# Spreading softmax sums over partitions by a DRAM round trip instead of wide transposes

## The reference, cut to what matters

```python
def _attn_ref(q, k, v, n_sink, window):          # 2 x 8 heads, 768 tokens, head_dim 64
    scores = scale * np.matmul(q, k.transpose(0, 1, 3, 2))
    keep = is_sink | in_window                   # 4 sinks, window 128
    scores = np.where(keep, scores, -1000000000.0)
    scores = scores - np.max(scores, axis=-1, keepdims=True)
    a = np.exp(scores)
    a = a / (np.sum(a, axis=-1, keepdims=True) + 1e-09)
    return np.matmul(a, v).astype(np.float32)
...
    x = np.ascontiguousarray(attn_out.transpose(0, 2, 1, 3)).reshape(B * S, H * D)
    x = _moe_ref(x=x, **moe_kwargs)              # silu(x w_gate) * (x w_val), times w_out
    return _moe2_ref(x=x, **moe2_kwargs)         # 8 experts, one for each token, skip gate
```

## Time and profile before

| | |
|---|---|
| median of 3 runs | 565.16 us (563.53 to 565.97) |
| the profiled execution | 564.08 us |
| its span, first to last instruction | 562.4 us |
| mean granted TensorE clock | 0.997 of 2.4 GHz |
| PE busy over the span | 545.3 us (97%) |
| attention, first instruction to the first product of the dense layer | 85.0 us |
| first 20 us to 40 us: PE, DVE, ACT, POOL busy | 20.00, 15.28, 14.55, 7.28 us |

### The profile page before, as it was taken

One profiled execution on the slowest core, in us unless ns is written; L12 is line 12 of the kernel. 1 busy time (PEld: TensorE's weight loads), 2 busy tenths in 40 slices (PEclk: granted clock), 3 DMA queues, 4 the chain that ended last, 5 costly groups with the idle time before them and its releaser, 6 DMA issues.

```text
span 562.4 us, 10755 instructions
## 1 busy us (share of the span) xinstructions
PE 545.3 (97%) x3830; PEld 454.0 (81%) x3830; DVE 237.4 (42%) x666; ACT 177.0 (31%) x421; POOL 102.6 (18%) x161
## 2 busy tenths in 40 slices
PE   7999999999999999999999999999989999999993
PEld 5777777888888888888888888888778888888882
DVE  5777771332323333232332444633641452445141
ACT  5777762121111212111133424322410330343030
POOL 7234457201111110100000010010211111111111
PEclk9999999999999999999999999999999999999998
DMA  8988522110011111000062112761267588396110
GB/s 234 276 272 233 163 80 79 57 56 21 36 56 56 56 56 56 0 0 1 0 249 106 56 53 74 276 251 57 100 200 273 187 331 314 123 332 228 43 29 28
DMA packets 28935, 71.67 MB, mean 127 GB/s; under 512 B 2833, under 2 KB 15121, under 8 KB 24801
## 3 DMA queue, kind: packets, MB, share of 16 engines
q1 hardware_dynamic: 25808, 62.82, 33.0%
q0 software_dynamic: 2560, 8.09, 4.5%
q10 hardware_dynamic: 528, 0.26, 0.2%
HBM read 61.11 MB, written 10.05 MB: 127 GB/s over the span
## 4 chain that ended last, share of the span: by engine, by line
PE 93%; DMA 2%; issue 1%; DVE 1%; POOL 1%; ACT 1%; POOLq 0%; DVEq 0%
PE bank L1518 13%; PE bank L1317 12%; PE bank L1315 12%; PE bank L1313 12%; PE bank L1390 6%; PE bank L1394 6%; PE bank L1392 6%; PE bank L1299 4%; PE bank L1530 4%; PE bank L1532 4%; PE bank L1531 4%; PE bank L1276 3%; PE bank L1255 3%; PE bank L1410 2%; PE bank L1269 1%
## 5 line engine op out<-in xcount | busy, mean ns | idle before, releaser
L1313 PE MATMUL bank<-x_hi,w_hi 128*128 128x512 f32 x288 | 112.2, 390 | 0.6 <-issue 0.6
L1317 PE MATMUL bank<-x_hi,w_lo 128*128 128x512 f32 x288 | 112.1, 389 | 0.0
L1315 PE MATMUL bank<-x_lo,w_hi 128*128 128x512 f32 x288 | 112.0, 389 | 0.0
L1518 PEld LDWEIGHTS bank<-xgT,w_sb 128*128 128x128 f32 x704 | 80.2, 192 | 2.3 <-issue 1.1
L1518 PE MATMUL bank<-xgT,w_sb 128*128 128x96 f32 x704 | 80.2, 275 | 1.0 <-ACT xgT L857 1.0
L1031 DVE TENSOR_TENSOR sig<-sig,bank 128x512 f32<-128x512 f32 x36 | 24.8, 688 | 128.1 <-ACT sig L759 128.1
L759 ACT ACTIVATE sig<-bank 128x512 f32<-128x512 f32 x36 | 21.5, 598 | 159.7 <-PE bank L1317 159.7
L1313 PEld LDWEIGHTS bank<-x_hi,w_hi 128*128 128x128 f32 x288 | 54.1, 188 | 12.2 <-issue 1.0
L1315 PEld LDWEIGHTS bank<-x_lo,w_hi 128*128 128x128 f32 x288 | 54.1, 188 | 11.3
L1317 PEld LDWEIGHTS bank<-x_hi,w_lo 128*128 128x128 f32 x288 | 54.0, 188 | 11.1
L1390 PE MATMUL bank<-wo_hi,hh_hi 128*128 128x512 f32 x132 | 53.6, 406 | 0.0
(11 more groups left out here) (173 smaller groups left out, 748.0 us busy)
## 6 DMA issues: line engine op xcount, KB each, us to landing
w_raw<-w SPq DMA_DIRECT2D x16, 1024.0 KB
w_sb<-w SPq DMA_DIRECT2D x16, 1024.0 KB, 7.6
w_raw<-w_gv SPq DMA_DIRECT2D x12, 512.0 KB, 3.5
va_sb<-v_long SPq DMA_DIRECT2D x10, 512.0 KB, 4.0
vb_sb<-v_tail SPq DMA_DIRECT2D x10, 320.0 KB, 5.6
k_sb<-kT SPq DMA_DIRECT2D x12, 256.0 KB, 6.2
wo_raw<-w_out SPq DMA_DIRECT2D x12, 256.0 KB, 3.6
out<-x SPq DMA_DIRECT2D x12, 256.0 KB, 2.1
```

The costliest lines, as they stand in the source:

```text
L1313: nc.tensor.matmul(ps[:, :], w_hi[:, u, a, k, :], x_hi[:, k, tok], start=(k == 0), stop=False)
L1315: nc.tensor.matmul(ps[:, :], w_hi[:, u, a, k, :], x_lo[:, k, tok], start=False, stop=False)
L1317: last = nc.tensor.matmul(ps[:, :], w_lo[:, u, a, k, :], x_hi[:, k, tok], start=False, stop=(k == KD - 1))
L1518: last = nc.tensor.matmul(ps, w1_sb[u][:, k, fc], xgT[:, k * ET:k * ET + ET], start=(k == 0), stop=(k == KD - 1))
```

## The change

The reciprocals stay 128x8. PE transposes them once into 8 partitions x 128 (8 rows of weights, one matmul). ACT copies that into `rsumT`. SP writes it to a DRAM tensor `sum_rows` and waits for it, and then reads it back with two transfers, each spreading 4 rows (2 KB) over 64 partitions, into `rbc_sb`, which has two halves now. X waits for these transfers (`rbc_in`). POOL's widening is gone. In the list, R moves from group B (after V of h 3) to group A (after its two T), X from group A to the group B that follows it, and Q from group A to the end of the group B before it. SP's `spread_sums(tile - 3)` stands between the loads of columns and of values.

```diff
--- before.py
+++ after.py
@@ -64,7 +64,7 @@
         for n in (g, g + 1):
             if n < PAIRS:
                 steps.append(("S", n // HP, n % HP, n))
-        for n in (g - 7, g - 6):
+        for n in (g - 9, g - 8):
             if 0 <= n < PAIRS and n % HP == HP - 1:
                 steps.append(("X", n // HP, None, n // HP))
         for n in (g - 3, g - 2):
@@ -72,17 +72,17 @@
                 steps.append(("T", n // HP, n % HP, psum_use))
                 turned[psum_use] = n
                 psum_use += 1
-                if n % HP == HP - 1:
-                    steps.append(("Q", n // HP, None, n // HP))
+        if g >= HP and (g - 3) % HP == HP - 1 and g - 3 < PAIRS:
+            steps.append(("R", (g - 3) // HP, None, psum_use))
+            psum_use += 1
         for n in (g - 5, g - 4):
             if 0 <= n < PAIRS:
                 tile, hp = divmod(n, HP)
                 steps.append(("V", tile, hp, None))
-                if hp == HP - 1:
-                    steps.append(("R", tile, None, psum_use))
-                    psum_use += 1
                 if tile in EARLY and hp == 1:
                     steps.append(("W", tile, None, tile - EARLY[0]))
+        if 0 < g <= PAIRS and (g - 1) % HP == HP - 1:
+            steps.append(("Q", (g - 1) // HP, None, (g - 1) // HP))
     v_use = itertools.count()
     return [(k, t, h, next(v_use)) if k == "V" else (k, t, h, n) for k, t, h, n in steps], turned
 
@@ -110,6 +110,7 @@
             return ctx.enter_context(nc.semaphore(name))
 
         expert_rows = nc.dram_tensor("expert_rows", (TRASH + P, ROW), F32).ap()
+        sum_rows = nc.dram_tensor("sum_rows", (NT, H, P), F32).ap()
 
 
         base = -(-nc.sbuf_base // 64) * 64
@@ -128,8 +129,8 @@
         scores_sb = place("scores_sb", (P, 4, SC), 0, 50.75)
         probsT = place("probsT", (P, TURNED, 4 * P), 0, 54.5)
         xT = place("xT", (P, 2, DM), 2, 0)
-        rbc_sb = place("rbc_sb", (P, DM), 2, 4)
-        rsum_wide = place("rsum_wide", (P, DM), 2, 6)
+        rbc_sb = place("rbc_sb", (P, 2, DM), 2, 4)
+        rsumT = place("rsumT", (P, 2, P), 2, 17)
         h_sb = place("h_sb", (P, NT, FT1, P), 0, 0)
 
 
@@ -275,7 +276,8 @@
         probs_ready = sem("probs_ready")
         pT_in_psum = sem("pT_in_psum")
         pT_by_act, pT_by_dve = sem("pT_by_act"), sem("pT_by_dve")
-        rsum_ready, rsum_spread = sem("rsum_ready"), sem("rsum_spread")
+        rsum_ready, rsum_out = sem("rsum_ready"), sem("rsum_out")
+        rbc_in = [sem("rbc_in0"), sem("rbc_in1")]
         pv_done = sem("pv_done")
         sums_step = sem("sums_step")
         silu_step = sem("silu_step")
@@ -401,16 +403,33 @@
                     sp.dma_start(va_sb[:, tile % 3, :, :], va[b, t - 1, :, :, :]).then_inc(v_in[t], 16)
                     sp.dma_start(vb_sb[0:TAIL, tile % 3, :, :], vb[b, t - 1, :, :, :]).then_inc(v_in[t], 16)
 
+            def spread_sums(tile):
+                use = next(n for kind, t, _, n in ORDER if kind == "R" and t == tile)
+                sp.wait_ge(pT_by_act, evacuated(use)[1])
+                sp.dma_start(sum_rows[tile, :, :], rsumT[0:H, tile % 2, :]).then_inc(rsum_out, 16)
+                sp.wait_ge(rsum_out, tile * 16 + 16)
+                if tile >= 2:
+
+                    sp.wait_ge(o_ready, tile - 1)
+                for u in range(2):
+                    sp.dma_start(rbc_sb[u * D:u * D + D, tile % 2, :],
+                                 sum_rows[tile, u * HP:u * HP + HP, :].rearrange("h q -> (h q)").unsqueeze(0)
+                                 .broadcast_to([D, DM])).then_inc(rbc_in[tile % 2], 16)
+
             load_columns(0)
             for tile in range(NT):
                 if tile + 1 < NT:
                     load_columns(tile + 1)
+                if tile >= 3:
+                    spread_sums(tile - 3)
                 load_values(tile)
                 if tile == QT - 1:
                     for f in range(2):
                         sp.dma_start(w_raw[:, f, :, :, :], w_gv[f, :, :, :, :]).then_inc(w_in[f], 16)
                         sp.dma_start(wo_raw[:, f, :], w_out[f, :, :]).then_inc(wo_in[f], 16)
                     sp.dma_start(wr_sb[:, :, :], w_route).then_inc(wr_in, 16)
+            for tile in range(NT - 3, NT):
+                spread_sums(tile)
             with if_wide(sp):
                 with sp.Fori(0, B) as b:
                     with sp.Fori(0, HP) as hp:
@@ -608,16 +627,11 @@
             make_mask(0)
             find_wide()
             for tile in range(NT):
-                if tile == QT - 1:
+                if tile == QT - 3:
                     copy_sinks(1)
-                pool.wait_ge(rsum_ready, tile + 1)
-                nc.gpsimd.tensor_copy(rsum_wide.rearrange("p (h c) -> p h c", h=H),
-                                      rsum[:, tile % 2, :].unsqueeze(2).broadcast_to([P, H, D])).then_inc(rsum_spread, 1)
-                if tile:
-                    split_x(tile - 1)
-                    if tile - 1 in EARLY:
-                        split_w(tile - 1 - EARLY[0])
-            split_x(NT - 1)
+                split_x(tile)
+                if tile in EARLY:
+                    split_w(tile - EARLY[0])
 
             with pool.Fori(0, FT1 // 2) as j:
                 for u in range(2):
@@ -726,9 +740,11 @@
                                          ).then_inc(pT_by_act, 1)
                 elif kind == "R":
                     a.wait_ge(pT_in_psum, n + 1)
-                    if tile:
-                        a.wait_ge(o_ready, tile)
-                    nc.scalar.activation(rbc_sb, pT_ps[n % 2][:, :], ACT.Copy).then_inc(pT_by_act, 1)
+                    if tile >= 2:
+
+                        a.wait_ge(rsum_out, (tile - 1) * 16)
+                    nc.scalar.activation(rsumT[0:H, tile % 2, :], pT_ps[n % 2][0:H, 0:P], ACT.Copy
+                                         ).then_inc(pT_by_act, 1)
                 elif kind == "W":
                     split_half(n // 2, n % 2, 16)
 
@@ -951,18 +967,18 @@
                                           ).then_inc(pT_by_dve, 1)
                 elif kind == "Q":
                     d.wait_ge(probs_ready, tile * H + H)
-                    nc.vector.tensor_scalar(rsum[:, tile % 2, :], sums[:, qt % 2, :], 1e-9, None, ALU.add
+                    nc.vector.tensor_scalar(rsum[:, tile % 2, :].rearrange("p (u h) -> p h u", u=2),
+                                            sums[:, qt % 2, :].rearrange("p (h u) -> p h u", u=2), 1e-9, None, ALU.add
                                             ).then_inc(sums_step, 1)
                     d.wait_ge(sums_step, tile + 1)
                     nc.vector.reciprocal(rsum[:, tile % 2, :], rsum[:, tile % 2, :]).then_inc(rsum_ready, 1)
                 elif kind == "X":
-                    use = next(m for k, t, _, m in ORDER if k == "R" and t == tile)
                     d.wait_ge(pv_done, LAST_V[tile] + 1)
-                    d.wait_ge(pT_by_act, evacuated(use)[1])
+                    d.wait_ge(rbc_in[tile % 2], tile // 2 * 32 + 32)
                     if tile >= 2:
 
                         d.wait_ge(xT_ready, tile - 1)
-                    nc.vector.tensor_tensor(xT[:, tile % 2, :], o_ps[tile % 2][:, :], rbc_sb, ALU.mult
+                    nc.vector.tensor_tensor(xT[:, tile % 2, :], o_ps[tile % 2][:, :], rbc_sb[:, tile % 2, :], ALU.mult
                                             ).then_inc(o_ready, 1)
 
             with if_wide(d):
@@ -1264,10 +1280,8 @@
                         by_act, count = evacuated(n - 2)
                         pe.wait_ge(pT_by_act if by_act else pT_by_dve, count)
                     if kind == "R":
-                        pe.wait_ge(rsum_spread, tile + 1)
-                        for hp in range(HP):
-                            last = nc.tensor.transpose(pT_ps[n % 2][:, hp * P:hp * P + P],
-                                                       rsum_wide[:, hp * P:hp * P + P], ident[:, :])
+                        pe.wait_ge(rsum_ready, tile + 1)
+                        last = nc.tensor.transpose(pT_ps[n % 2][0:H, 0:P], rsum[:, tile % 2, :], ident[:, :])
                     else:
                         pe.wait_ge(probs_ready, tile * H + h * 2 + 2)
                         for u in range(2):
```

## The result

The changed kernel takes 594.28 us (median of 4 runs, 592.10 to 594.98), the kernel before 564.91 beside it. The ratio is 1.0527, 95% interval 1.0503 to 1.0551. The direction was forecast, the size was not: 579.0 was the number, 573 to 587 its range.

A forecast was written before the change was run, and what follows sets the result against it. PE was taken as the bound, busy all of 20 us in attention. Tiles' extra times, mainly R waiting for ACT's copy, summed to 14.1 us on 564.08, giving 578.2 (579.2 beside the median), range 573 to 587.

The forecast's parts named there:

- R's wait for ACT: In group A, PE's R waits for ACT's copy of h 3, ending 3.45 us in; group A takes 4.79 instead of 2.97.
- the sum: Over attention, the changes in tile times add up to 14.1 us more, giving 578.2, or 579.2 beside the median.
- The saving of 0.4 us for the single transpose: On PE, R falls from 0.59 to 0.2 us, giving back 0.4 us a tile, 4.8 us by itself.
- Q and X move on DVE into group B: DVE ends 4.02 us after group B's start, shifting the chain to ACT's copy by 0.25; group A takes 5.04 us.
- the paragraph on POOL: POOL is busy 7.28 of 20 us and nobody waits for its copy, so removing it is worth nothing.
- 0 to 4 us there and take 0: At tile 3, the sums' write queues behind tile 5's values and 1.5 MB of weights; cost put at 0.
- The rival that put the whole trip late: SP's chain of write, reads and loads sets the pace, 7.5 to 9 us a tile, about 586; 25 in 100.
- The end: After the last R, the trip takes 9.2 to 10.3 us against 11.8 available: hidden, 1.5 us to spare.
- the rival with the shorter chain: R waits, but DVE's shift is 0 and X hidden; a tile pays 1.1 us, about 575; 15 in 100.
- From there everything is shifted and nothing is longer: Sign to look for: first dense product comes at 99, and everything behind it is only shifted.

The follow-up runs named there:

- The order alone: Kernel before with the changed kernel's attention order, double rbc_sb, but still four transposes and POOL's spreading copy, no DRAM trip: 584.48 us, ratio 1.0353.
- the last variant: Kernel before, without DRAM trip, with R at the head of group A, Q in group B before the copies, X in group A: 566.83 us, ratio 1.0039.

## Why the forecast was right in direction and half in size

The step that was to decide, R's wait for ACT, came as forecast. Three terms of the sum failed: Q on DVE was priced at 0.32 us and took 1.11, the clock behind R's wait had no term, and the DRAM trip was taken at 0 and cost 3 to 5 us.

**What PE waits for: right.** R in group A waits 11 times for ACT's copy of h 3. The order alone gives a tile of 8.08 us against 8.17 and 14.0 us against the sum's 14.1, and moving the copy to DVE takes 10.8 us of it away. The saving of 0.4 us for the single transpose holds too: 0.20 in place of 0.59.

**"Q and X move on DVE into group B": mis-sized.** The term priced Q at 0.32 us from the earlier trace rows. It measured 1.11. R's waits add up to 21.5 us, against 17.8 where the order stands alone and Q is short: 3.7 us. The mistake is in the paragraph on POOL: "the removal is worth nothing". POOL's copy had waited for Q and kept `x_lo` behind it. Moving Q brought DVE and POOL together, and removing the copy took the guard away. The Trainium skill (SBUF — State Buffer, SBUF: two separate sides) says that DVE and GpSimd share one pair of ports, an exclusive lock that a GpSimd instruction, or a DVE instruction in a mode with two ports, holds for its whole length, so that the other blocks. The trace agrees for Q's first half, which ends with POOL's subtraction in every tile where it is long, and takes 0.17 us where it is moved away. The two copies just before it, which read PSUM, take 1.28 us beside POOL's work, as in the earlier trace rows. That it is the lock, and nothing else the two share, was not tried.

**The clock: not in the sum at all.** V and S behind R were priced at the durations of before, where PE never stood for long. In the late tiles the account above gives 1.46 us, and filled waits gave 1.31 back. With the four late tiles that is 5 to 6 us at PE, of which the kernel with those four waits filled had 3.75 at the first product. The changed kernel shows four more such stretches, three of them here by PE's granted clock:

```profile
22.00:27.00 5.00, 5.00 (x80) 3.83 (x76) 3.45 (x12) 2.03 (x9) 1.37 (x2) 0.66 0.91 263
40.00:44.00 4.00, 4.00 (x54) 3.07 (x55) 1.41 (x9) 1.27 (x6) 0.00 (x0) 0.57 0.73 193
57.00:60.00 3.00, 2.79 (x27) 2.45 (x28) 2.97 (x12) 0.39 (x2) 1.88 (x2) 0.55 0.44 127
```

The fourth is 50 to 54 us, 0.57, and the one at 57 lasts to 61, also 0.57. Together they lack 5 x 0.34 + 3 x 4 x 0.43 = 6.9 us of full clock. Most of this is no separate loss. The four late stretches and those at 40 and 50 us came behind waits of 2.30 to 2.36 us, which Q had made so long, and the one at 57 behind V's 2.29 us for X. But the first came behind an R with a wait near the forecast's own:

```profile
21.53 0.27 PE L1284 MATMUL bank<-ident,rsum 128*8 128x128 f32 x1 [1.62 <-ACT probsT L739]
```

Waits of 1.82 and 1.54 us, at R of tiles 0 and 2, had no such stretch behind them, nor had the 11 waits in the order alone. So the length of one wait doesn't settle it, and even the forecast's wait could cost clock, which the sum put at nothing without a word.

**The DRAM trip: "0 to 4 us there and take 0".** It was nearer the far end: 3 to 5 us at the first product, of which the medians show 2.7, not clear of their noise. The rival that put the whole trip late, 586, had the mechanism for it, and said that PE's slower pace speaks against. Both held. In the changed kernel the trip is hidden in most tiles, because R's wait slows them. Take that wait away and the trip is the bound, at 109.68 instead of 90.21. Its estimate of 7.5 to 9 us a tile is what that kernel shows (R at 18.06 and 44.04, 8.66 a tile).

Sum: 14.0 (order) + 3.7 (Q) + 5.8 (clock, 4 x 1.46) + 5.4 (trip) = 28.9 against 30.6 measured at the first product. The four more slow stretches (above) are not in it, and would add up to 6.9 us, 35.8 in all. The parts were measured in different kernels and overlap: the kernel without the trip's wait has two slow stretches fewer, so its 5.4 us hold some of the clock's. So this is an account and no proof, and how much each overlap holds is open.

**Smaller slips, none of which moves the forecast.** In "The end", 6.3 less 0.57, twice, is 11.5 us and not 11.8, so the spare was 1.2 us. In the rival with the shorter chain a tile pays 4.79 + 2.97 - 6.73 = 1.03 us, not 1.1.

**What follows attention.** "From there everything is shifted and nothing is longer" held: 476.9 us behind the first product against 477.4.

## What to carry to other kernels

When a step is moved to another place on its engine, price it with what the neighbour engines do at that time, and look at what the removed instruction was holding back: a copy that nobody waits for can be the guard between two engines. When a forecast puts a wait on TensorE, price what follows the wait once at full and once at half clock. And ask of each hidden transfer by how much it is hidden, for it is the next bound as soon as the one in front of it goes.

## What the runs showed of the hardware

- TensorE stood for 2.36 us a tile and then worked at a granted clock of 0.50 (1.2 GHz) for about 3 us. Behind waits of 1.55 to 1.82 us, 11 of them in the new order alone, the clock was 1.00 throughout; behind one of 1.62 us in the changed kernel it fell to 0.50, and behind another of 2.04 us in the last variant.
- A DVE operation of 128x8 took 0.95 us instead of 0.16 next to a POOL subtraction of 1.28 us, and ended 0.02 us after it.
- The write of 4 KB kept its queue waiting up to 6.6 us from SyncE and up to 6.5 from POOL, while columns and values were loaded, and 0.94 us from SyncE when no load was in flight.
